# Seven drains on GpSimd: one among the experts, one in each window of the feed-forward

## The chip, the core and the metric

The kernel runs on one core of a Trainium2 chip. The metric is the device time of one execution in microseconds (us), as a median over runs. The core has five engines that matter here, each with its own stream of instructions: TensorE (PE; PEld is its weight load), VectorE (DVE), ScalarE (ACT), GpSimd (POOL) and SyncE (SP). They are tied together by semaphores alone, and the order of each stream is the order in which the kernel's code was written.

## The reference

Three layers in a row on 3072 tokens of width 384, all in float32: an attention-like scan over chunks, a mixture of 8 experts with one expert for each token, and a feed-forward with a leaky activation.

```python
def _moe_ref(x, w_gate, w_output_gate, w1, w2):
    logits = x @ w_gate
    e_idx = np.argmax(logits, axis=1)
    ...
    for e in range(E):                       # E = 8
        mask = e_idx == e
        h = np.maximum(x[mask] @ w1[e], 0.0)  # 384 -> 1024
        ye = h @ w2[e]                        # 1024 -> 384
        out[mask] = gate_w[mask, None] * eom[mask, e, None] * ye

def _moe2_ref(x, w_in, w_out):
    h = x @ w_in                              # 384 -> 2048
    g = np.maximum(0.01 * h, h)
    return (g @ w_out).astype(np.float32)     # 2048 -> 384
```

## The kernel before, in words

The scan takes roughly the first 300 us. It leaves the tokens sorted by expert in DRAM, and a small table that says for each block of 128 tokens which expert it has.

**How a float32 product is made.** Each operand of a matrix product is split into a leading part (rounded to the type fp32r) and a trailing part (the rest), and three products are summed in PSUM: leading by leading, and the two mixed ones. So each set of weights and each activation must be split before TensorE can use it.

**The experts** (about 300 to 590 us). TensorE works through the blocks of 128 tokens in a loop: layer 1 (L2060), transposes (L2036, L2070), layer 2 (L2082). The weights of an expert come in two halves, `w1` and `w2`, each 128 x 3072 elements (1536 KB), into the two halves of one staging tile `stage`. GpSimd does the splitting in `split(lot, i, ...)`: it waits until half `i` of the load has landed, and for `i == 0` also until TensorE is through with the expert before last, whose room the new weights take. It writes the leading part (L1843), waits for that on its own semaphore, writes the trailing part (L1845), waits for that too, and only then issues the load of the next lot into the same half of `stage` (L1848). There are ten lots: the eight experts, `w_out` and `w_in` of the feed-forward. Lot 0 is split elsewhere; `split` runs for lots 1 to 9. TensorE waits for the two halves of an expert's weights before that expert's first block.

**The feed-forward** (about 593 us to the end). It runs over 6 windows of 512 tokens. In a window, f counts 16 slices of the 2048 hidden elements. For each f TensorE makes the hidden slice (`ff1`, L2102, 9 matmuls), ScalarE takes a hundredth of it (L1927), VectorE the larger of the two (L1991), ScalarE its leading part (L1930), and GpSimd its trailing part (`trail(w, f)`, L1871), after which TensorE may multiply it with `w_out` (`ff2`, L2115, 12 matmuls). TensorE's order is ff1 of slice f + 2, then ff2 of slice f, so that a slice has two turns of TensorE's work in which to pass through the other engines. `act_f` has two buffers: VectorE waits for `trail` of slice f before it writes slice f + 2. After the last slice of a window GpSimd does the first two slices of the next window, and then issues four indirect DMAs that scatter the finished rows (L1877).

Of the kernel before, what the change touches and what calls it, by code (L numbers as in the profile page):

```python
# [23 lines left out]
E = 8  # L24
# [13 lines left out]
FT2 = F2 // P  # L38
# [1650 lines left out]
def experts_then_feed_forward(nc, ctx, sem, sb, bank, ident, ids, stage, masks_at, wm, wbase, w_out_r, ys, moe_w, w_in,  # L1689
# [65 lines left out]
    def at(eng, base, g, lo, hi):  # L1755
        return eng.value_load(table[0:1, bass.ds(base + g, 1)], min_val=lo, max_val=hi)
# [10 lines left out]
    def windows(eng, body):  # L1767
        for w in range(NW):
            body(w, w < NW - 1)
# [58 lines left out]
    def layers_pool(pool):  # L1828
        pool.wait_ge(s_split0, 2)
        pool.sem_inc(s_wh, 2)  # L1830
        pool.wait_ge(s_table, 1)
        pool.wait_ge(s_slots, 1)
        lots = [moe_w[e] for e in range(E)] + [w_out, w_in]

        def split(lot, i, lead, trail, done):

            u = 2 * lot + i
            half = stage[:, i * WE:(i + 1) * WE]
            pool.wait_ge(*((s_stage[i], 32) if lot == 1 else (s_more[i], 16 * (lot - 1))))
            if i == 0 and done is not None:  # L1840

                pool.wait_ge(s_p2, done)
            pool.tensor_scalar(lead, half, 1.0, 0.0, ALU.mult, ALU.add).then_inc(s_ws, 1)  # L1843
            pool.wait_ge(s_ws, u - 1)
            pool.tensor_tensor(trail, half, lead.bitcast(F32), ALU.subtract).then_inc(s_wh, 1)  # L1845
            pool.wait_ge(s_wh, u + 1)
            if lot + 1 < len(lots):
                pool.dma_start(half, lots[lot + 1][:, i * WE:(i + 1) * WE]).then_inc(s_more[i], 16)  # L1848

        def sort_ids(tiles):  # L1850
            for t in tiles:
                pool.indirect_dma_start(
                    out=sorted_ids, out_offset=bass.IndirectOffsetOnAxis(ap=slot_of[:, t:t + 1].bitcast(U32), axis=0),
                    in_=token[:, t:t + 1], in_offset=None).then_inc(s_sorted, 16)

        for e in range(1, E):
            done = at(pool, T_CUM, e - 2, 1, NBMAX) if e >= 2 else None
            for i in range(2):
                split(e, i, wm[:, e % 2, i, :], wm[:, e % 2, 2 + i, :], done)
            if 2 <= e < 2 + B:  # L1860
                sort_ids(range((e - 2) * NCH // B, (e - 1) * NCH // B))
        for i in range(2):
            split(E, i, w_out_r[:, 0, i * WE:(i + 1) * WE], w_out_r[:, 1, i * WE:(i + 1) * WE], None)
        done = at(pool, T_CUM, E - 2, 1, NBMAX)
        for i in range(2):
            split(E + 1, i, w_in_r[:, 0, i * WE:(i + 1) * WE], w_in_r[:, 1, i * WE:(i + 1) * WE], done)

        def trail(w, f):
            pool.wait_ge(s_gh, w * FT2 + f + 1)
            a = act_r[f % 4]  # L1870
            pool.tensor_tensor(a[:, 1, :], act_f[f % 2][:, :], a[:, 0, :].bitcast(F32),  # L1871
                               ALU.subtract).then_inc(s_gl, 1)

        def scatter(w):
            for j in range(TW):
                pool.wait_ge(s_o, TW * (w + 1) + j + 1)
                pool.indirect_dma_start(  # L1877
                    out=out, out_offset=bass.IndirectOffsetOnAxis(ap=ids[:, TW * w + j:TW * w + j + 1].bitcast(U32), axis=0),
                    in_=o_sb[j][:, :], in_offset=None).then_inc(s_out[j], 16)

        def body(w, more):
            for f in range(2, FT2):
                trail(w, f)
            if more:
                for f in range(2):
                    trail(w + 1, f)
            scatter(w)

        for f in range(2):
            trail(0, f)  # L1890
        pool.wait_ge(s_ids, 16)
        windows(pool, body)

    def layers_scalar(act):
# [317 lines left out]
```

## Time and profile before

| what | us |
|---|---|
| median of 3 runs | 1013.23 (1013.14 to 1015.47) |
| the profiled execution, its own time | 1014.68 |
| span of that execution, first to last instruction | 1012.7 |
| TensorE busy with matmuls | 941.1 (93% of the span) |
| GpSimd busy | 505.5 (50%) |
| ScalarE busy | 453.9 (45%) |
| VectorE busy | 415.9 (41%) |

The busy times are read first: one engine is near full, the others are at about half. A share over the whole span says little about one stage, so the stretches of the three stages are to be read apart, and for each engine what ended its idle time. The time of an instruction that does no work on data, such as a wait or a drain, isn't counted as busy; it can only be seen as idle time between its neighbours. The profiled execution's time is 1.98 us more than its span; what lies around the span is not in the profile.

### The profile page before, as it was taken

How to read it: one execution, taken by the hardware profiler on the slowest of the kernel's cores; microseconds unless marked ns; L12 is line 12 of the kernel's file. 1: busy time of each engine (PE TensorE's matmuls, PEld its weight loads, DVE VectorE, ACT ScalarE, POOL GpSimd, SP SyncE). 2: the span in 40 equal slices, each digit the busy share in tenths (PEclk: the TensorE clock that was granted, in tenths of full speed). 3: DMA queues.
4: the chain of work that ended last, by engine and by line, in shares of the span. 5: the costliest groups of instructions: out<-in, count | busy, mean ns of one | idle time of the engine just before them, and what ended most of it. 6: DMA issues, size and time to landing. Idle time of an engine off the chain costs nothing.

```text
span 1012.7 us, 17328 instructions
## 1 busy us (share of the span) xinstructions
PE 941.1 (93%) x5836; PEld 832.5 (82%) x5837; DVE 415.9 (41%) x742; ACT 453.9 (45%) x772; POOL 505.5 (50%) x429
## 2 busy tenths in 40 slices
PE   1899999999838999999999999999999999999995
PEld 0677778887736999998998989999999999999995
DVE  6698998998844233233232322212112121121110
ACT  7899888897612232232222333333333333333322
POOL 4134565565556568568839943342342433433433
PEclk9999999999978999999999999999999999999998
DMA  4542463430252343343534520010010100000000
GB/s 149 166 134 80 124 214 103 112 110 17 100 171 96 106 163 107 103 163 104 155 114 163 186 57 17 16 39 16 9 39 17 39 16 17 32 1 1 32 1 32
DMA packets 47190, 84.04 MB, mean 83 GB/s; under 512 B 23812, under 2 KB 36376, under 8 KB 44568
## 3 DMA queue, kind: packets, MB, share of 16 engines
q1 hardware_dynamic: 40984, 48.59, 16.0%
q0 software_dynamic: 6144, 34.65, 9.7%
q8 instruction: 37, 0.61, 0.3%
q14 instruction: 25, 0.20, 0.1%
HBM read 65.80 MB, written 17.38 MB: 82 GB/s over the span
## 4 chain that ended last, share of the span: by engine, by line
PE 72%; ACT 10%; issue 6%; DVE 6%; POOL 4%; SPq 1%; DMA 1%; POOLq 0%; DVEq 0%; ACTq 0%
PE bank L2102 20%; PE bank L2115 19%; PE bank L2060 11%; PE bank L2082 10%; POOL wm L1845 3%; PE bank L2070 2%; PE bank L1136 1%; PE bank L1119 1%; PE bank L1138 1%; POOL wm L1843 1%; PE bank L1096 1%; DVE neglog L848 1%; PE bank L1178 1%; PE bank L2036 1%; PE bank L1106 1%
## 5 line engine op out<-in xcount | busy, mean ns | idle before, releaser
L1871 POOL TENSOR_TENSOR act_r<-act_f,act_r 128x512 fp32r<-128x512 f32 x96 | 124.4, 1296 | 260.5 <-ACT act_r L1930 257.8
L2115 PE MATMUL bank<-w_out_r,act_r 128*128 128x384 f32 x1152 | 217.7, 337 | 0.3 <-POOL act_r L1871 0.3
L2102 PE MATMUL bank<-x,w_in_r 128*128 128x512 f32 x864 | 216.7, 395 | 0.0
L2115 PEld LDWEIGHTS bank<-w_out_r,act_r 128*128 128x128 f32 x1152 | 204.8, 188 | 8.8 <-POOL act_r L1871 0.6
L1991 DVE TENSOR_TENSOR act_f<-bank,small 128x512 f32<-128x512 f32 x96 | 66.4, 692 | 292.7 <-ACT small L1927 275.2
L2102 PEld LDWEIGHTS bank<-x,w_in_r 128*128 128x128 f32 x864 | 159.6, 188 | 29.4
L1927 ACT ACTIVATE small<-bank 128x512 f32<-128x512 f32 x96 | 57.4, 598 | 191.5 <-PE bank L2102 191.4
L2060 PE MATMUL bank<-wm,x_tr 128*128 (+1 forms) x522 | 129.1, 401 | 4.0 <-POOL wm L1845 1.7
L2082 PE MATMUL bank<-wm,h_tr 128*128 (+1 forms) x696 | 128.6, 339 | 0.7 <-DVE h_tr L1975 0.7
L2082 PEld LDWEIGHTS bank<-wm,h_tr 128*128 128x128 f32 x696 | 120.1, 188 | 1.0 <-issue 1.0
L2060 PEld LDWEIGHTS bank<-wm,x_tr 128*128 128x128 f32 x522 | 97.6, 191 | 24.8 <-issue 5.0
L1845 POOL TENSOR_TENSOR wm<-stage,wm 128x3072 fp32r<-128x3072 f32 x14 | 95.3, 6808 | 1.2
L1930 ACT ACTIVATE act_r<-act_f 128x512 fp32r<-128x512 f32 x96 | 60.7, 632 | 72.8 <-DVE act_f L1991 72.8
L1907 ACT ACTIVATE h_tr<-bank 128x512 fp32r<-128x512 f32 x58 | 31.6, 596 | 120.5 <-PE bank L2070 120.5
L1843 POOL TENSOR_SCALAR wm<-stage 128x3072 fp32r<-128x3072 f32 x14 | 38.9, 2780 | 71.3 <-PE bank L2082 56.3
L1902 ACT ACTIVATE h<-bank 128x512 f32<-128x512 f32 x58 | 31.5, 596 | 71.4 <-PE bank L2060 71.4
L1119 PE MATMUL bank<-q_t,k_t 96*128 96x128 f32 x384 | 56.2, 291 | 4.5 <-ACT q_t L696 2.7
L1981 DVE COPY y_b<-bank 128x384 f32<-128x384 f32 x29 | 16.2, 558 | 95.1 <-PE bank L2082 80.4
L1136 PE MATMUL bank<-ident,qr 128*96 128x128 f32 x192 | 46.8, 282 | 7.3 <-DVE qr L911 7.3
L1119 PEld LDWEIGHTS bank<-q_t,k_t 96*128 96x128 f32 x384 | 48.3, 197 | 6.1 <-ACT q_t L696 4.2
L1966 DVE CAST x_tr<-bank 128x384 fp32r<-128x384 f32 x30 | 16.7, 558 | 80.5 <-PE bank L2036 80.5
L1975 DVE TENSOR_TENSOR h_tr<-bank,h_tr 128x512 fp32r<-128x512 f32 x58 | 37.4, 686 | 21.3 <-ACT h_tr L1907 21.0
(193 smaller groups left out, 1378.1 us busy)
## 6 DMA issues: line engine op xcount, KB each, us to landing
stage<-moe_w POOLq DMA_DIRECT2D x12, 1536.0 KB, 7.0
qkv_in<-in_qkv SPq DMA_DIRECT2D x24, 576.0 KB, 5.5
a_in<-in_a SPq DMA_DIRECT2D x11, 768.0 KB, 5.3
stage<-moe_w SPq DMA_DIRECT2D x4, 1536.0 KB
x_b<-x_sorted SPq DMA_DIRECT2D x30, 193.0 KB
y_sorted<-y_b SPq DMA_DIRECT2D x29, 192.0 KB
xg<-y_sorted SPq DMA_DIRECT2D x24, 192.0 KB, 2.4
stage<-w_out POOLq DMA_DIRECT2D x2, 1536.0 KB, 7.1
```

The lines of the kernel that those rows point to most:

```text
L1119: last = pe.matmul(sc_bank[:, a * C:(a + 1) * C], k_t[h][:, a * C:(a + 1) * C], q_t[h][:, a * C:(a + 1) * C], start=True, stop=True)
L1136: pe.transpose(qt_bank[0:2 * D, a * C:(a + 1) * C], qr[n % 2][:, head, :, :].rearrange("p c d -> p (c d)"), ident[:, :])
L1843: pool.tensor_scalar(lead, half, 1.0, 0.0, ALU.mult, ALU.add).then_inc(s_ws, 1)
L1845: pool.tensor_tensor(trail, half, lead.bitcast(F32), ALU.subtract).then_inc(s_wh, 1)
L1871: pool.tensor_tensor(a[:, 1, :], act_f[f % 2][:, :], a[:, 0, :].bitcast(F32), ALU.subtract).then_inc(s_gl, 1)
L1927: act.activation(small[f % 2][:, :], h_bank[f % 2][:, :], ACT.Copy, scale=0.01).then_inc(s_c, 1)
L1930: act.activation(act_r[f % 4][:, 0, :], act_f[f % 2][:, :], ACT.Copy).then_inc(s_gh, 1)
L1991: dve.tensor_tensor(act_f[f % 2][:, :], h_bank[f % 2][:, :], small[f % 2][:, :], ALU.max).then_inc(s_g, 1)
L2060: last = pe.matmul(hid_bank[j][:, :], x_tr[:, xp, t * P:(t + 1) * P], wmf[:, part_of(base, wp * WE + t * F1 + j * 512, 512)], start=(t == ...
L2082: last = pe.matmul(ye_bank[:, 0:W], h_tr[:, hp, t * P:(t + 1) * P], wmf[:, part_of(base, wp * WE + t * W, W)], start=(t == 0 and n == 0), ...
L2102: last = pe.matmul(h_bank[f % 2][:, :], w_in_r[:, wp, t * F2 + f * P:t * F2 + (f + 1) * P], window_part(w, xp)[:, t, :], start=(t == 0 and ...
L2115: last = pe.matmul(o_bank[j][:, 0:W], a[:, ap, j * P:(j + 1) * P], w_out_r[:, wp, f * W:(f + 1) * W], start=(f == 0 and n == 0), stop=(f = ...
```

## The change

`drain()` puts an instruction into GpSimd's stream that holds the stream until the engine's earlier instructions have ended. It moves no data and releases nobody. The change adds seven: one in `split`, for lot 6 (the seventh expert's weights) and its second half, between the wait for the trailing part and the issue of the load of lot 7's second half; and one in each of the 6 windows, between `trail(w, 8)` and `trail(w, 9)`. In the built program GpSimd has 582 instructions for 575 before; the numbers of the other engines are the same, and nothing else changes its place. At the first drain the wait for the trailing part of the split (count 14 of its semaphore) is held by the drain now, and the load behind it has no wait of its own. The drains in the windows carry no wait on a semaphore.

```diff
@@ in split(lot, i, lead, trail, done) @@
             pool.tensor_tensor(trail, half, lead.bitcast(F32), ALU.subtract).then_inc(s_wh, 1)
             pool.wait_ge(s_wh, u + 1)
+            if lot == E - 2 and i == 1:
+                pool.drain()
             if lot + 1 < len(lots):
                 pool.dma_start(half, lots[lot + 1][:, i * WE:(i + 1) * WE]).then_inc(s_more[i], 16)
@@ in body(w, more) @@
             for f in range(2, FT2):
                 trail(w, f)
+                if f == FT2 // 2:
+                    pool.drain()
             if more:
                 for f in range(2):
                     trail(w + 1, f)
```

## Rows read from the trace of the kernel before

**Rows 1.** The page's head and first part: busy us, share, instructions.
```profile
span 1012.7 us, 17328 instructions
PE 941.1 (93%) x5836; PEld 832.5 (82%) x5837; DVE 415.9 (41%) x742; ACT 453.9 (45%) x772; POOL 505.5 (50%) x429
```

**Rows 2.** Busy time by stretch (columns in the first row), all engines.
```profile
core 0: us, PE busy (x) PEld busy (x) DVE busy (x) ACT busy (x) POOL busy (x), PEclk, DMA share, GB/s
480.00:548.00 68.00, 66.99 (x372) 61.04 (x373) 21.00 (x36) 19.13 (x36) 46.82 (x19) 1.00 0.43 133
548.00:593.00 45.00, 44.21 (x249) 40.35 (x250) 14.77 (x26) 12.50 (x25) 39.93 (x11) 1.00 0.46 158
593.00:997.00 404.00, 404.00 (x2052) 365.67 (x2051) 78.11 (x117) 135.07 (x232) 142.57 (x115) 1.00 0.07 21
```

**Rows 3.** Timeline, GpSimd, lots 6 and 7: start, duration, work [idle before <-releaser].
```profile
499.99 0.62 POOL L1848 DMA_DIRECT2D stage<-moe_w  x1 [0.30 <-POOL wm L1845]
500.65 2.77 POOL L1843 TENSOR_SCALAR wm<-stage 128x3072 fp32r<-128x3072 f32 x1
503.50 6.83 POOL L1845 TENSOR_TENSOR wm<-stage,wm 128x3072 fp32r<-128x3072 f32 x1
510.63 0.62 POOL L1848 DMA_DIRECT2D stage<-moe_w  x1 [0.30 <-POOL wm L1845]
527.28 2.77 POOL L1843 TENSOR_SCALAR wm<-stage 128x3072 fp32r<-128x3072 f32 x1 [16.04 <-PE bank L2082]
...
537.87 2.78 POOL L1843 TENSOR_SCALAR wm<-stage 128x3072 fp32r<-128x3072 f32 x1
540.73 6.80 POOL L1845 TENSOR_TENSOR wm<-stage,wm 128x3072 fp32r<-128x3072 f32 x1
```

**Rows 4.** Timeline, TensorE, first block of the last expert.
```profile
547.87 4.36 PE L2060 MATMUL bank<-wm,x_tr 128*128 x18 [0.84 <-POOL wm L1845]
```

**Rows 5.** The tile `stage`, 300 to 600 us: durations in ns min/median/max, and its loads.
```profile
L1845 POOL TENSOR_TENSOR wm<-stage,wm x14: 6789/6807/6829, 315.9 to 540.7; 128x3072 fp32r<-128x3072 f32 x14
...
DMA to landing us min/median/max: 6.5/6.9/7.9
```

**Rows 6.** Timeline, first window, around slices 8 and 9, several engines.
```profile
627.12 1.30 POOL L1871 TENSOR_TENSOR act_r<-act_f,act_r 128x512 fp32r<-128x512 f32 x1 [3.24 <-ACT act_r L1930]
...
631.31 1.30 POOL L1871 TENSOR_TENSOR act_r<-act_f,act_r 128x512 fp32r<-128x512 f32 x1 [2.89 <-ACT act_r L1930]
...
633.00 2.18 PEld L2115 LDWEIGHTS bank<-w_out_r,act_r 128*128 128x128 f32 x12
...
637.52 2.18 PEld L2115 LDWEIGHTS bank<-w_out_r,act_r 128*128 128x128 f32 x12
...
638.59 0.69 DVE L1991 TENSOR_TENSOR act_f<-bank,small 128x512 f32<-128x512 f32 x1 [1.64 <-ACT small L1927]
```

**Rows 7.** Timeline, last window, around slices 8 and 9.
```profile
968.17 1.30 POOL L1871 TENSOR_TENSOR act_r<-act_f,act_r 128x512 fp32r<-128x512 f32 x1 [2.89 <-ACT act_r L1930]
...
972.36 1.30 POOL L1871 TENSOR_TENSOR act_r<-act_f,act_r 128x512 fp32r<-128x512 f32 x1 [2.89 <-ACT act_r L1930]
...
978.24 1.83 PEld L2115 LDWEIGHTS bank<-w_out_r,act_r 128*128 128x128 f32 x10
```

**Rows 8.** Timeline, the last slice: GpSimd, then the weight load it releases.
```profile
997.48 1.28 POOL L1871 TENSOR_TENSOR act_r<-act_f,act_r 128x512 fp32r<-128x512 f32 x1 [2.89 <-ACT act_r L1930]
998.82 3.10 PEld L2115 LDWEIGHTS bank<-w_out_r,act_r 128*128 128x128 f32 x18 [0.61 <-POOL act_r L1871]
```

**Rows 9.** Timeline, GpSimd: the first window's last scatter, and the second window's slice 9.
```profile
670.86 0.96 POOL L1877 DMA_INDIRECT out<-o_sb,ids  x1 [0.30 <-issue]
...
699.65 1.30 POOL L1871 TENSOR_TENSOR act_r<-act_f,act_r 128x512 fp32r<-128x512 f32 x1 [2.89 <-ACT act_r L1930]
```

**Rows 10.** DMA issues by line: KB each, median us to landing.
```profile
out<-o_sb,ids POOLq DMA_INDIRECT x24, 2.6
```

**Rows 11.** Timeline, GpSimd in the scan: like instructions of unlike length.
```profile
267.93 0.20 POOL L551 TENSOR_TENSOR sel<-sel,whole_sum 128x4 f32<-128x4 f32 x1
268.21 3.27 POOL L552 TENSOR_TENSOR den<-sel,whole_sum 128x4 f32<-128x4 f32 x1
...
276.66 0.96 POOL L560 DMA_INDIRECT x_sorted<-x_ring,pos  x1 [0.30 <-issue]
277.92 4.02 POOL L560 DMA_INDIRECT x_sorted<-x_ring,pos  x1 [0.30 <-issue]
```

**Rows 12.** Timeline, the step from the experts to the feed-forward.
```profile
582.32 6.76 POOL L1845 TENSOR_TENSOR w_in_r<-stage,w_in_r 128x3072 fp32r<-128x3072 f32 x1
...
592.90 6.32 PE L2102 MATMUL bank<-x,w_in_r 128*128 128x512 f32 x27
```

## The prediction, made before the changed kernel was run

> **What bounds the kernel now.** I read the page's head first: TensorE is busy for 941.1 of 1012.7 us, GpSimd for 505.5 [rows 1]. Then the busy time by stretch, because a share over the span mixes three stages. In the feed-forward, from 593 to 997 us, TensorE is busy for 404.00 of 404.00 us, and GpSimd for 142.57 [rows 2]. In the two stretches of the experts behind the first new drain TensorE is idle for 68.00 - 66.99 = 1.01 us and for 45.00 - 44.21 = 0.79 us [rows 2]. So everything that comes behind the first drain, up to the last slices, is bound by TensorE, and a change that touches GpSimd alone can do two things: nothing, or make TensorE wait. The reader is to see in these rows that GpSimd's idle time in the feed-forward (404.00 - 142.57 = 261.43 us) is not a loss; it is the cover under which the drains lie.
>
> Then the timeline of GpSimd around the places of the drains, to see how long the idle time is right behind each, what ends it, and how much later GpSimd could be before TensorE noticed.
>
> **The change, part by part.** It removes nothing and moves nothing. It adds seven instructions on GpSimd that hold that stream until earlier work has ended. So its cost is one unknown, the time X that a drain takes once the work before it has ended, set against the slack at each of two kinds of place.
>
> *The drain at lot 6.* The trailing part of the split starts at 503.50 and takes 6.83 us, so it ends at 510.33; the load of lot 7's second half is issued 0.30 us later, at 510.63, since it waits for that same instruction [rows 3]. The engine is idle at that moment already, so the drain has nothing to wait out. Behind it stand the issue of the load, and then the split of lot 7, which starts at 527.28 after 16.04 us of idle time that TensorE ends: it was waiting for room, for the last block of an expert before [rows 3]. Two bounds follow. GpSimd itself gets late only if X is over 16.04 us. The load must have landed when the second half is split, at 537.87; issued at 510.63 and landing after at most 7.9 us [rows 5] it is there at 518.5, so it may be issued 19.3 us later. The smaller one decides: X up to 16.0 us costs nothing here. This place has to be checked with care because what comes behind is on the path: TensorE starts the last expert's first block at 547.87, after 0.84 us of waiting for the end of that very split [rows 4], which ends at 540.73 + 6.80 = 547.53 [rows 3]. Once the 16 us were used up, each further us would be paid in full.
>
> *The drains in the windows, six of them.* In the first window slice 8 is split from 627.12 to 628.42 [rows 6]. The drain then stands between it and the split of slice 9, which starts at 631.31 and was waiting for ScalarE for 2.89 us [rows 6]. Up to X = 2.89 us the drain only takes the place of that wait, and nothing on any engine moves. Beyond that slice 9 gets late, but TensorE needs it only at 637.52, where the weight load of its ff2 starts; slice 8's, already split before the drain, stands at 633.00 [rows 6]. From the end of a split to the weight load that it releases it takes 998.82 - (997.48 + 1.28) = 0.06 us, as the last slice shows, where TensorE did wait [rows 8]. So slice 9 may start as late as 637.52 - 0.06 - 1.30 = 636.16, which is 7.74 us behind the end of slice 8's split. VectorE, which needs the buffer of slice 9 back for slice 11, starts that at 638.59 [rows 6], later still. In the last window the same sum gives 978.24 - 0.06 - 1.30 - (968.17 + 1.30) = 7.41 us [rows 7]. The idle time ahead of slice 9 is 2.89 us in the first, the second and the last window [rows 6, 7, 9]; I take the four windows between to be like the first. So a drain costs the kernel nothing up to 7.4 us, and above it 6 times what is over.
>
> *How long is X?* No row of before shows a drain on GpSimd amid work. The nearest row is the wait of GpSimd on its own last instruction, 0.30 us, ahead of the load [rows 3]. That wait is there already at lot 6, and the drain takes it over, so there the low end is zero. A drain has no data to move, so I see no gain from it and no end below zero. The high end: were the drain also to wait for what GpSimd's queue of transfers still has in flight, it could take as long as the slowest load, 7.9 us [rows 5]. But little is in flight: at lot 6 the load of the first half was issued at 499.99 and is there by 507.9 at the latest, before 510.33 [rows 3, 5], and in the windows the last scatter, issued at 670.86 for the first of them and landing after 2.6 us, lies over 20 us ahead of the next drain, which stands just before slice 9 at 699.65 [rows 9, 10]. I take X = 0.3 us, the nearest row.
>
> The sum at X = 0.3 us: 0 at lot 6 (0.3 of 16.0), 6 x 0 in the windows (0.3 of 2.89, and of 7.4). At the high end, X = 7.9: 0 at lot 6, and 5 x (7.9 - 7.74) + (7.9 - 7.41) = 1.3 us in the windows. From the profiled execution's own time, 1014.68 us (span 1012.7 and 1.98 around it), that makes 1014.68, at most 1016.0. The profiled execution lies 1.45 us above the median of the runs, 1013.23, and within their spread of 1013.14 to 1015.47; carried over to the median the forecast is 1013.3 us.
>
> A rule that could speak against this: GpSimd's instructions run as software, and the Trainium skill (GPSIMD Engine Reference, section 2.1 Instruction dispatch) says that the first call of a freshly loaded routine pays some 6 us for loading its code, with no instruction in the profile to show it. No row here shows such a load behind a drain. If each drain led to one, slice 9 would start at 628.42 + 6 = 634.4 by that figure, still ahead of 636.16, so the estimate by the page and the estimate by the row give the same time; the page's figure only uses up most of the cover.
>
> **The rivals.**
>
> *A, slower: the drain is dear.* Should a drain on GpSimd take as long as a whole split of a half, 2.77 + 6.83 = 9.60 us [rows 3], it would pass the cover in all six windows: 5 x (9.60 - 7.74) + (9.60 - 7.41) = 11.5 us, hence 1013.23 + 11.5 = 1024.7 us. It would show as TensorE's weight load for slice 9 waiting for GpSimd, once in each window. The point from which it decides is X = 7.4 us, and 7.9 us for a loss over 0.3% is not enough: 3.04 us need 6 x 0.5, so X of about 8.2 us. For it speaks only that no row prices a drain. Against it: nothing on GpSimd that does so little takes so long; the longest of its single instructions here, with 128 x 3072 elements, takes 6.83 us [rows 3].
>
> *B, slower: a hiccup of GpSimd's stream at a bad place.* In the scan two small instructions take 3.27 and 4.02 us where their like take 0.20 and 0.96, some 3.1 us more each [rows 11]. What they are I can't read here; they may hang on where an instruction stands in the stream, and the change moves all that follow by one to seven places. In the feed-forward such a hiccup would be hidden. Between 527.28 and 547.53 it would not: TensorE waits for the end of lot 7's split, and 3.1 us there are 3.1 us in the end, 1016.3 us. At the start of the feed-forward there is 592.90 - (582.32 + 6.76) = 3.8 us between the last split and the first product [rows 12], so there it would be hidden too. Against it: the 14 trailing parts of the experts' weights take 6.789 to 6.829 us, none longer [rows 5], wherever they stand in the stream.
>
> *C, faster.* A gain needs an idle TensorE that the drains fill. Behind the first drain there are 1.01 + 0.79 us of idle time up to 593 [rows 2], and none of it is ended by something that a drain brings forward. Even all of it, 1.8 us, would be within 0.3%: 1011.4 us.
>
> *D, the drain does nothing.* If the stream holds for no time at all the forecast is the same, 1013.2 us. It can't be told from the forecast by the time, only by the gaps on GpSimd.
>
> **How the numbers follow.** The measurement can tell from no change what is over 0.3%, here 3.04 us. The forecast together with D has a chance of 0.92, C 0.02, A 0.03, and B 0.03. The predicted time is the forecast's, 1013.3 us. Its range comes from the spread of the runs before and the bounds of X: from 1012.4, a little under the lowest run, to 1015.4, where the highest run lies; the high end of X on top of the median, 1013.23 + 1.3 = 1014.5, is within. A and B lie outside and have 6 in 100. Of faster by over 0.3% I give 0.03 (C, and a shift between two measurements), of slower 0.05 (A and those of B that exceed the bound), of within 0.3% 0.92.
>
> **What would show it.** Right: the gap between the splits of slices 8 and 9 is still 2.89 us and ended by ScalarE, in all six windows; the split of lot 7 still starts when TensorE's block ends; TensorE is busy for the whole of the feed-forward. At lot 6 the gap of 0.30 us ahead of the load may grow, and its growth is X. Wrong: a gap at slice 9 over 2.89 us that ScalarE doesn't end prices the drain above the cover's first part, and TensorE waiting for GpSimd at slice 9 is rival A. A longer instruction or gap on GpSimd from 527 to 548 is rival B. The forecast falls altogether if a stage ahead of the first drain, where nothing was changed, differs between the two profiles by more than the whole difference in time: then the cause isn't in the drains' places at all.

## The result: 0.6% faster, and where it came from

| | before | changed |
|---|---|---|
| median of 9 runs, us | 1014.38 | 1010.25 |
| lowest, us | 1013.14 | 1007.71 |
| ratio (95% interval) | | 0.994 (0.9915 to 0.9966) |
| profiled execution, its own time, us | 1014.68 | 1014.22 |
| its span, us | 1012.7 | 1012.2 |

One of the nine executions of the changed kernel took 1897 us and is left out of the ratio. The quotient of the two medians is 0.996. The forecast was 1013.3 us with a range of 1012.4 to 1015.4; the time is below it, by a gain that I had given 3 in 100.

The two profiled executions differ by only 0.5 us, and that is a trap: a kernel's executions differ by some us in the scan, ahead of the change (apart from the one that is left out, the spans of the changed kernel's other executions are 1005.7 to 1010.2 us). So the two spans are cut at three points that both have: the first product of the first block of the experts (L2060, now L2064), the first product of the feed-forward (L2102, now L2106), and the end of GpSimd's last split (L1871, now L1873).

| stretch, us | before | changed | difference |
|---|---|---|---|
| start to the first block | 307.78 | 311.92 | +4.14 |
| first block to the feed-forward | 285.12 | 285.57 | +0.45 |
| feed-forward, to the end of the last split | 405.86 | 405.86 | 0.00 |
| from there to the end of the span | 13.94 | 8.85 | -5.09 |

The first row lies ahead of every drain of the change. In the eleven kernels below, none of which is changed there, that point lies anywhere from 305.18 to 309.04. The 311.92 is later still; this execution is the slowest of the changed kernel's eight, and why it was late stays open. The 0.45 us of the second row are within the spread too: in the nine kernels below that have no drain behind lot 6 among the experts, that stretch takes 284.3 to 285.8 us. The last row is the effect. No instruction was added in that stretch. The timeline of GpSimd at the end, first of before, then of the changed kernel (start, duration, line, work, [idle before]):

```profile
core 0 of [0], span 1012.7 us
...
1000.41 0.98 POOL L1877 DMA_INDIRECT out<-o_sb,ids  x1 [1.65 <-ACT o_sb L1922]
...
1004.23 0.96 POOL L1877 DMA_INDIRECT out<-o_sb,ids  x1 [0.30 <-issue]
```

```profile
core 0 of [0], span 1012.2 us
...
1005.00 0.98 POOL L1879 DMA_INDIRECT out<-o_sb,ids  x1 [1.65 <-ACT o_sb L1926]
...
1008.82 0.96 POOL L1879 DMA_INDIRECT out<-o_sb,ids  x1 [0.30 <-issue]
```

Behind the end of the last issue of a scatter there were 1012.7 - 1005.19 = 7.51 us; now there are 1012.2 - 1009.78 = 2.42 us. I call this stretch the tail. The landing doesn't fill it: a scatter lands 2.6 us behind the start of its issue [rows 10], here at 1004.23 + 2.6 = 1006.8, and that is 5.9 us before the end of the span.

What fills it is in the trace. The `--source` view of L151, the line that opens the block around all engines' streams (`with nc.Block()`), shows a drain of GpSimd in the kernel before (duration in ns, then the start of the first and of the last in us), with SyncE beside it:

```profile
core 0 of [0], span 1012.7 us
...
L151 POOLq DRAIN  x1: 9651/9651/9651, 1002.8 to 1002.8; - x1
...
L151 SPq DRAIN  x1: 7/7/7, 1007.0 to 1007.0; - x1
L151 SPq EVENT_SEMAPHORE  x1: 17/17/17, 1012.6 to 1012.6; - x1
```

The same view of the changed kernel:

```profile
core 0 of [0], span 1012.2 us
...
L151 POOLq DRAIN  x1: 4190/4190/4190, 1007.4 to 1007.4; - x1
```

A drain's record can open while the instructions ahead of it still run, so its end is what counts. In before it ends at 1002.80 + 9.65 = 1012.45, which is 7.27 us behind the last issue. SyncE is through at 1007.0 and, like the other engines, has one semaphore event left, which comes at 1012.6, behind GpSimd's drain. In the changed kernel the drain ends at 1011.58, which is 1.80 us behind the last issue and 0.2 us behind the landing of the last scatter.

Now the places of the drains. The timeline of the changed kernel at lot 6, which answers to [rows 3], and at slices 8 and 9 of the first window, which answer to [rows 6]:

```profile
507.29 6.80 POOL L1845 TENSOR_TENSOR wm<-stage,wm 128x3072 fp32r<-128x3072 f32 x1
519.54 0.62 POOL L1850 DMA_DIRECT2D stage<-moe_w  x1 [5.46 <-issue]
531.88 2.77 POOL L1843 TENSOR_SCALAR wm<-stage 128x3072 fp32r<-128x3072 f32 x1 [11.73 <-PE bank L2086]
...
631.71 1.30 POOL L1873 TENSOR_TENSOR act_r<-act_f,act_r 128x512 fp32r<-128x512 f32 x1 [3.24 <-ACT act_r L1934]
635.90 1.30 POOL L1873 TENSOR_TENSOR act_r<-act_f,act_r 128x512 fp32r<-128x512 f32 x1 [2.89 <-ACT act_r L1934]
```

The gap ahead of the load is 5.46 us for 0.30: the drain took some 5 us on an engine that had nothing left to do (its record is 4.89 us long and opens 0.03 us behind the end of the split). The next split still starts when TensorE gives up the room, after 11.73 us of idle time. The gaps ahead of slice 9 are 2.89 us in all six windows, as before; the records of those drains end 0.4 to 0.5 us behind the split of slice 8. The busy time by stretch has the feed-forward as it was, against [rows 2]:

```profile
593.00:997.00 404.00, 403.81 (x2051) 365.86 (x2052) 78.52 (x119) 133.93 (x230) 141.93 (x115) 1.00 0.07 21
```

(In this execution the feed-forward started at 597.49, so the stretch holds the last 4.5 us of the experts too.) So 5.2 us were spent under cover at lot 6, and 5.1 us were saved at the end.

### The profile page after: what moved, and what is told of

Same layout as the page of the kernel before. It is cut to its first block, busy times and chain, and to the rows that moved or that the text cites. A ratio compares the mean times of both kernels' runs of the same rounds, so it can differ in the third digit from the quotient of the medians.

```text
span 1012.2 us, 17335 instructions
## 1 busy us (share of the span) xinstructions
PE 944.0 (93%) x5836; PEld 835.1 (83%) x5837; DVE 415.1 (41%) x742; ACT 454.0 (45%) x772; POOL 505.8 (50%) x429
## 4 chain that ended last, share of the span: by engine, by line
PE 72%; ACT 9%; issue 6%; DVE 6%; POOL 4%; SPq 1%; DMA 1%; POOLq 0%; DVEq 0%; ACTq 0%
PE bank L2106 20%; PE bank L2119 19%; PE bank L2064 11%; PE bank L2086 10%; POOL wm L1845 3%; PE bank L2074 2%; PE bank L1136 1%; PE bank L1119 1%; PE bank L1096 1%; POOL wm L1843 1%; PE bank L1138 1%; DVE neglog L848 1%; PE bank L1164 1%; PE bank L1178 1%; PE bank L2040 1%
## 5 line engine op out<-in xcount | busy, mean ns | idle before, releaser
L1873 POOL TENSOR_TENSOR act_r<-act_f,act_r 128x512 fp32r<-128x512 f32 x96 | 124.4, 1296 | 260.5 <-ACT act_r L1934 258.1
L2106 PE MATMUL bank<-x,w_in_r 128*128 128x512 f32 x864 | 216.7, 395 | 0.0
L2106 PEld LDWEIGHTS bank<-x,w_in_r 128*128 128x128 f32 x864 | 159.6, 188 | 29.4
L2064 PE MATMUL bank<-wm,x_tr 128*128 (+1 forms) x522 | 129.6, 402 | 3.9 <-POOL wm L1845 1.7
L2064 PEld LDWEIGHTS bank<-wm,x_tr 128*128 128x128 f32 x522 | 97.9, 192 | 25.0 <-issue 5.0
```

The costliest lines, as they stand in the source:

```text
L2064: last = pe.matmul(hid_bank[j][:, :], x_tr[:, xp, t * P:(t + 1) * P], wmf[:, part_of(base, wp * WE + t * F1 + j * 512, 512)], start=(t == ...
L2106: last = pe.matmul(h_bank[f % 2][:, :], w_in_r[:, wp, t * F2 + f * P:t * F2 + (f + 1) * P], window_part(w, xp)[:, t, :], start=(t == 0 and ...
```

## The experiments

The program's own drain at the end of GpSimd's stream, behind the last scatter, is in both kernels. So the first idea was that a drain there is dear when none has run for long. Two theories about why came to stand against each other: **A**, it depends on the time, or on what else GpSimd has run, since the last drain (code that has to be fetched again); **B**, a drain pays for each DMA that GpSimd has issued since the last one. In before there are 88 of them: 24 scatters of the scan, 16 loads in `split`, 24 writes of the sorted ids and 24 scatters of the output.

All edits are shown against the kernel before, `...` standing for lines left out. Each run goes by the short name e1 to e11 from here on. Ratios are against runs of before on the same chip.

### One part of the change alone

`e1_lot6_only`: the first drain of the change alone.

```diff
+            if lot == E - 2 and i == 1:
+                pool.drain()
```

> Only the drain at lot 6 is kept; the six in the windows are gone. In the profile after, the gap ahead of the load was 5.46 us instead of 0.30, and from the end of the last scatter's issue to the end of the span it was 2.4 us instead of 7.5. Theory 1 (the program has a drain of its own at the end of GpSimd's stream, a drain costs some 5 us when none has run for long, and a drain shortly before makes it cheap): this drain lies 490 us before the end, with 96 splits of activations and 28 indirect DMAs between; if it is the last drain that counts, the tail is back at 7.5 us and the time at that of before (1013 to 1014 us). Theory 1b (one drain anywhere behind the scan is enough): the tail is 2.4 us and the time is that of after, about 5 us below before. Theory 2 (rival: the measured gain is a difference in the scan between runs, nothing that drains do): tail and time as in before, and so in every kernel of this set.

`e2_windows_only`: the six in the windows alone.

```diff
+                if f == FT2 // 2:
+                    pool.drain()
```

> Only the six drains in the windows are kept; lot 6 is as before. Theory 1: the tail is 2.4 us, the time about 5 us below before, as after. The first window's drain is the first for long and should cost some 5.2 us, so slice 9 of the first window starts about 5.2 us behind the end of slice 8 instead of 2.89, and later windows show 2.89; TensorE does not wait, since it has 7.4 us. Theory 1b: the same. Theory 2: no difference in time from before beyond the noise, tail 7.5 us.

`e3_last_window_only`: of these, the last alone.

```diff
+                if w == NW - 1 and f == FT2 // 2:
+                    pool.drain()
```

> One drain alone, in the last window behind slice 8, some 35 us before the end. Theory 1: the gap ahead of slice 9 of the last window grows from 2.89 to about 5.2 us, the tail falls from 7.5 to 2.4 us, and the time is about 5 us below before, as with all seven. A variant of theory 1 (it needs two or more drains to make the next one cheap) would leave the tail at 7.5 us. Theory 2: as before.

Measured, 6 runs each: e1 1009.74 us, ratio 0.9955 (0.9942 to 0.9967); e2 1010.03, ratio 0.9947 (0.9933 to 0.9961); e3 1009.16, ratio 0.9943 (0.993 to 0.9955); before 1014.41. Each part alone brings nearly the whole gain. The rival that it is a difference of the scan is out, and so is the idea that only a recent drain counts: e1's lies 490 us ahead of the end. (That the time since the last drain decides is hard to hold from here on.) The tails are 3.11, 2.12 and 2.12 us.

The gaps are the more telling. The timeline of e1 at lot 6:

```profile
514.13 0.62 POOL L1850 DMA_DIRECT2D stage<-moe_w  x1 [5.46 <-issue]
```

That of e2, slices 9 and 10 of the first window, and that of e3 in the last window:

```profile
634.21 1.29 POOL L1871 TENSOR_TENSOR act_r<-act_f,act_r 128x512 fp32r<-128x512 f32 x1 [5.42 <-issue]
635.88 1.29 POOL L1871 TENSOR_TENSOR act_r<-act_f,act_r 128x512 fp32r<-128x512 f32 x1 [0.37 <-ACT act_r L1932]
```

```profile
976.92 2.54 POOL L1871 TENSOR_TENSOR act_r<-act_f,act_r 128x512 fp32r<-128x512 f32 x2 [7.05 <-ACT act_r L1932]
```

In e3 I had expected about 5.2 us. The drain took 7.05, and there are 84 DMAs before it, 20 more than the 64 before e2's: 1.63 us for 20. TensorE didn't notice either: from the first product of the feed-forward to the end of the last split it is 405.86 us in all three, within 0.01.

### A drain behind every half

`e4_every_half`: the drain in `split` without a condition, 18 in all, none in the windows.

```diff
             pool.wait_ge(s_wh, u + 1)
+            pool.drain()
```

> A drain behind every split of a half, lots 1 to 9 (18 drains), ahead of each load; none in the windows. Each gap ahead of a load prices one drain: 0.30 us is the gap without. Between the two halves of a lot lie one issue of a load and two arithmetic instructions; between lots 2 to 5 and the next one lie also six indirect DMAs and a load of a register from the table. Theory 1 as a matter of code that GpSimd has to fetch again once other routines have pushed it out: the first drain costs about 5.2 us, the others little, and those after indirect DMAs perhaps 5 us again. A rival (a drain has to work off what has gathered since the last one, such as the bookkeeping of the transfers that GpSimd issued): the cost follows the number of DMAs since the last drain, greatest at the first (24 indirect DMAs of the scan), middling after six, least after one.

Its timeline at the loads of lots 1 (both halves) and 3 (both halves):

```profile
324.13 0.63 POOL L1849 DMA_DIRECT2D stage<-moe_w  x1 [2.66 <-issue]
335.17 0.61 POOL L1849 DMA_DIRECT2D stage<-moe_w  x1 [0.68 <-POOL wm L1845]
...
393.27 0.61 POOL L1849 DMA_DIRECT2D stage<-moe_w  x1 [1.20 <-issue]
404.28 0.60 POOL L1849 DMA_DIRECT2D stage<-moe_w  x1 [0.68 <-POOL wm L1845]
```

The first gap is 2.66 us with 24 DMAs before it, not 5.2; with 7 since the last drain (a load and six writes of ids) the gap is 1.20, with one 0.66 to 0.68. That is 0.087 us for each of six, and 0.086 for each of the 17 between 7 and 24. Theory A expected about 5.2 us at the first; the number of DMAs orders all gaps seen so far. (There was one execution of this kernel, 1011.67 us. Its tail is 2.87 us, but from the first block to the feed-forward it takes 288.03 us instead of some 285: eighteen drains among the experts are not all under cover.)

### The last drain far from the end, and at the wrong place

`e6_lot1_only`: one drain, behind the first half of lot 1.

```diff
+            if lot == 1 and i == 0:
+                pool.drain()
```

> One drain alone, behind the first half of lot 1. Theory B (a drain pays for the DMAs that GpSimd issued since the last drain, about 0.08 us each): 24 indirect DMAs lie before it, so its gap is 2.66 us as in the run with a drain at every half; 64 lie between it and the program's own drain at the end (16 loads, 24 and 24 indirect). From the last issue of a scatter to the span's end it took 7.5 us with 88, 3.1 with 28, and 2.1 to 2.4 with 4, so 0.073 us for each between the first two: about 5.7 us with 64, and the time 1.8 us below before (ratio 0.998). Theory A with one drain anywhere being enough: that tail under 3.1 us and the time about 5 us below (ratio 0.995). Theory A by elapsed time (the last drain 690 us before the end against 490 with lot 6 alone): between these two, with no number of its own.

Measured: 1012.30 us against 1014.37, ratio 0.9983 (0.9973 to 0.9993), 12 runs; gap 2.67, tail 1011.8 - 1006.28 = 5.52 us. Theory B's numbers were 0.998 and 5.7. (The expectation counts 28 DMAs behind the drain of e1; it is 29: 5 loads and 24 scatters.)

`e7_before_last_scatter`: one drain, behind the last split of all, ahead of the last four scatters.

```diff
+                if w == NW - 1 and f == FT2 - 1:
+                    pool.drain()
```

> One drain alone, between the last split of all and the four last scatters. Theory B: it pays for 84 DMAs, about 7.05 us as in the last window, but here on the path: the first of the last scatters starts about 7.1 us behind the end of the last split instead of 1.65, 5.4 us later; the tail behind the scatters falls from 7.5 to between 2.1 and 2.4 us, 5.2 less; the time is that of before within 0.5 us (ratio 0.9995 to 1.0005). So the gain would be a matter of where the cost lies, not of drains. If drains saved something by themselves, the ratio would be about 0.995 here too.

Its timeline at the end:

```profile
core 0 of [0], span 1011.5 us
...
995.67 1.28 POOL L1871 TENSOR_TENSOR act_r<-act_f,act_r 128x512 fp32r<-128x512 f32 x1 [2.88 <-ACT act_r L1932]
1004.65 0.98 POOL L1877 DMA_INDIRECT out<-o_sb,ids  x1 [7.70 <-issue]
...
1008.47 0.96 POOL L1877 DMA_INDIRECT out<-o_sb,ids  x1 [0.30 <-issue]
```

The scatter comes 7.70 us behind the split instead of 1.65, and the tail is 2.07 us: +6.05 and -5.44. Measured: 1015.68 us against 1014.37, ratio 1.002 (1.0007 to 1.0034), 12 runs. I had expected no change within 0.5 us, and it is slower. The scatter comes 0.6 us later than I had reckoned (7.70 for 7.1); that is about the lower end of the interval, 0.7 us, and what the rest is stays open. The drain itself took no longer than in e3. Its record, by the line of the drain, first here, then in e3:

```profile
L1885 POOLq DRAIN  x1: 8279/8279/8279, 995.6 to 995.6; - x1
```

```profile
L1885 POOLq DRAIN  x1: 8294/8294/8294, 968.5 to 968.5; - x1
```

It ends 6.96 us behind the split ahead of it in both; the scatter is issued 0.74 us behind that end, where e3's split starts 0.09 us behind it. The kind of thing is as expected: the same work is done, only in the open. A drain saves nothing by itself.

### More DMAs

`e8_more_dmas_one_row` and `e9_more_dmas_128_rows`: the drain of e3, and 24 more DMAs issued by GpSimd, which write to a spare tensor (1 row of 4 bytes; in e9 128 rows). SyncE waits for them at the end, with its waits for the scatters. `e10_more_dmas_no_drain`: the DMAs of e8, and no drain.

```diff
...
+                if w < 4 and f in (4, 6, 8, 10, 12, 14):
+                    k = 6 * w + f // 2 - 2
+                    pool.dma_start(spare[k, 0:1, :], pos[0:1, 0:1]).then_inc(s_sorted, 16)
+                if w == NW - 1 and f == FT2 // 2:   # not in e10
+                    pool.drain()
```

> The one drain in the last window, as in the run with it alone (gap ahead of slice 9 there 7.05 us with 84 DMAs since the start), and 24 more DMAs issued by GpSimd in the first four windows, six in each, that write one row of 4 bytes each to a spare tensor. Theory B by number of DMAs: 24 x 0.0815 = 2.0 us more, gap about 9.0 us. Theory B by rows or descriptors moved: no more than 0.1 us more. Theory A (time or other code since the last drain): 7.05 us.

> As the one before, with 128 rows of 4 bytes in each of the 24 added DMAs. By number of DMAs: about 9.0 us again. By rows: the 24 x 128 rows are as many as those of 24 scatters of 128 rows; the 20 scatters between the first window's gap of 5.42 and the last's of 7.05 cost 1.63 us, so again about 9.0 us. With the one-row kernel this tells number from rows: both 9.0, number; 7.05 and 9.0, rows.

The timelines at slice 9 of the last window, e8, then e9:

```profile
976.08 2.51 POOL L1874 TENSOR_TENSOR act_r<-act_f,act_r 128x512 fp32r<-128x512 f32 x2 [9.01 <-issue]
```

```profile
976.11 2.51 POOL L1874 TENSOR_TENSOR act_r<-act_f,act_r 128x512 fp32r<-128x512 f32 x2 [9.01 <-issue]
```

(One execution of each, 1008.32 and 1008.40 us.) The gap is 9.01 us in both, where 9.0 had been worked out from the number: 1.96 us over e3 for 24 DMAs, 0.082 us each, and not a hundredth of a us for 127 rows more in each. Time and other work since the start are as in e3. Theory A is out, and so is a cost by rows. These gaps also pass the cover that the prediction had reckoned for a drain in the last window, 7.41 us: the feed-forward up to the last split now takes 407.27 us (e8) instead of 405.86, so 1.41 us are paid, where 9.01 - 7.41 gives 1.60.

> No drain is added at all; GpSimd issues 24 more DMAs of one row of 4 bytes in the first four windows. Theory B: the program's own drain at the end pays for 112 instead of 88, so the tail from the last scatter's issue to the end of the span grows from 7.5 us by 24 x 0.0815 = 2.0 to about 9.5 us, and the time is 2 us above before (ratio 1.002), although the added DMAs themselves lie under TensorE's work, some 50 us and more before the end. Rival (the tail of before is something else that a drain happens to shorten, not the program's own drain counting DMAs): tail 7.5 us, ratio 1.000.

Measured: 1015.70 us against 1014.47, ratio 1.002 (1.0007 to 1.0034), 11 runs. The timeline of GpSimd's last scatter in it:

```profile
core 0 of [0], span 1014.0 us
...
1003.60 0.96 POOL L1880 DMA_INDIRECT out<-o_sb,ids  x1 [0.30 <-issue]
```

The tail is 1014.0 - 1004.56 = 9.44 us; expected were 9.5. The kernel gets slower by DMAs that lie over 100 us before its end, and the feed-forward itself is unchanged (405.84 us). This ties the tail to the program's own drain: no other drain stands behind a DMA in this kernel, and its record has grown from 9.65 to 11.61 us, by 1.96 us:

```profile
L151 POOLq DRAIN  x1: 11614/11614/11614, 1002.2 to 1002.2; - x1
```

### What a drain costs by itself, and the cover behind lot 7

`e5_eight_in_a_row`: at lot 6, eight drains instead of one.

```diff
+            if lot == E - 2 and i == 1:
+                for _ in range(8):
+                    pool.drain()
```

> Eight drains in a row at lot 6, none elsewhere. With one the gap was 5.46 us, with 59 DMAs issued by GpSimd before it. Theory B (a drain pays about 0.08 us for each DMA that GpSimd issued since the last drain, and little for itself): the seven behind the first have none to pay for, so the gap is 5.46 us plus seven times a fixed cost, at most 0.3 us each (with one DMA since the last drain the gap was 0.68, 0.38 over that without a drain), hence 5.6 to 7.6 us. If each drain paid for all DMAs of the program so far, drained or not, the gap would be over 40 us.

Its timeline at that load:

```profile
514.50 0.61 POOL L1851 DMA_DIRECT2D stage<-moe_w  x1 [5.90 <-issue]
```

The gap is 5.90 us for 5.46 with one: (5.90 - 5.46) / 7 = 0.06 us for a drain that has no DMA to pay for (the records of the seven are 0.034 us long). A drain does not pay again for DMAs that an earlier one has paid for. (One execution, 1008.82 us.)

`e11_lot7_only`: one drain, one lot later than in e1 (`lot == E - 1 and i == 1`).

> One drain alone, one lot later: behind the second half of lot 7, ahead of the load of w_out's second half. 61 DMAs lie before it, so the gap is 5.46 + 2 x 0.08 = 5.6 us, 5.3 more than 0.30. GpSimd has no idle time from there to the end of lot 9 to take it up, so lots 8 and 9 are 5.3 us late; the last split then ends 5.3 us later, and TensorE, which had 3.8 us to spare there, starts the feed-forward 1.5 us later (by the end of the last split). The tail has 27 DMAs to pay for: about 3.0 us instead of 7.5. Sum: 1.5 - 4.5 = -3.0 us, ratio about 0.997, against 0.9955 with the drain at lot 6. Should the place not matter, the ratio is 0.9955 here too.

Its timeline, GpSimd at the load and TensorE at the start of the feed-forward:

```profile
551.60 0.59 POOL L1850 DMA_DIRECT2D stage<-w_out  x1 [5.61 <-issue]
...
593.15 6.38 PE L2104 MATMUL bank<-x,w_in_r 128*128 128x512 f32 x27 [1.67 <-POOL w_in_r L1845]
```

Measured: 1011.25 us against 1014.47, ratio 0.9972 (0.9963 to 0.9981), 11 runs; tail 2.99 us. The gap is 5.61 for 5.6 expected, TensorE waits for GpSimd for 1.67 us for 1.5, and the ratio is the 0.997 of the sum. So the cover is real, and its end is where the timeline of before puts it.

### All of it in one table

| drain at | DMAs since the last drain | gap or tail, us | from the end of the work ahead to the end of the drain's record, us |
|---|---|---|---|
| a load (gap 0.30 without): e4, e4, e4, e1, e11 | 1, 7, 24, 59, 61 | 0.68, 1.20, 2.66, 5.46, 5.61 | 0.16, 0.66, 2.07, 4.93, 5.09 |
| a split in a window: e2, e3, e8 | 64, 84, 108 | 5.42, 7.05, 9.01 | 5.32, 6.96, 8.92 |
| ahead of the last scatters: e7 | 84 | 7.70 | 6.96 |
| the program's end (tail): changed and e3, e4, e11, e1 | 4, 24, 27, 29 | 2.42 and 2.12, 2.87, 2.99, 3.11 | 1.80, 2.62, 2.76, 2.83 |
| the same: e6, before, e10 | 64, 88, 112 | 5.52, 7.51, 9.44 | 5.30, 7.27, 9.23 |

From 1 to 61 DMAs at a load the gap grows by 4.93 us, 0.082 for each; in the windows by 0.082; in the tail from 64 to 112 by 0.082. The last column puts the places on one line: with 64 DMAs it has 5.32 us in a window and 5.30 at the end. At the program's end the cost flattens out below some 30: 1.80 us with 4 DMAs, where a window of the changed kernel has 0.4. There the last scatter is still under way, since it lands 1.6 us behind the end of its issue. The drain ends 0.20, 1.03, 1.16 and 1.24 us behind that landing with 4, 24, 27 and 29 DMAs, so it looks as if a part of its work waited for the landing; no run was made to test that. So the change takes the program's own drain from 88 DMAs to 4.

No version beats the changed one: e2 and e3 are as fast within the intervals, e3 with one drain instead of seven. Of the tail of 2.1 us that they leave, the last scatter's landing takes 1.6 us.

## Why the prediction was wrong

**The step that failed is the first: "a change that touches GpSimd alone can do two things: nothing, or make TensorE wait"**, and with it "I see no gain from it and no end below zero". It holds up to the last slices, as the prediction says itself, and then the prediction leaves the rest out. Rival C sums the idle time of TensorE "behind the first drain" up to 593 us and with the feed-forward's none; the 13.94 us from the last split to the end of the span are in no sum. In them GpSimd is what is waited for. Its last scatter has landed at 1004.23 + 2.6 = 1006.8 [rows 10], and the span ends 5.9 us later. Those 5.9 us that nothing explained were the lower bound that the sum should have had, and would have made the low end about 1007.3 us, which holds the measured 1010.25. The reason given against a gain was that a drain has no data to move. That it may do work that another drain would do later was not considered, though the program ends with one. The trace of before even had a price: the document said ahead of the prediction that a drain can only be seen as idle time between its neighbours, but the view of L151 has its record, 9.65 us long. The measured gain passes all of rival C, whose 1.8 us already lay outside the stated range.

**X, the time of a drain, was mis-sized**: 0.3 us was taken, from a wait on GpSimd's own last instruction, and the drain at lot 6 made that gap 5.16 us longer (4.89 us is its record). The high end of 7.9 us was worked out from a different mechanism, transfers in flight; it holds for this change, but only by accident: at lot 6 nothing was in flight that could last so long, and with 108 DMAs the gap was 9.01. Something of that mechanism shows only at the program's end, where the drain with 4 DMAs ends 0.2 us behind the last landing.

**The cover was right.** Lot 6 had 16.0 us, of which the drain used 5.2: the split of lot 7 still starts when TensorE gives up the room. A window has 7.4 to 7.7 us: 7.05 us in e3 cost nothing, 9.01 in e8 cost 1.41. Behind lot 7, 3.8 us [rows 12]: e11 is late by 1.67. That the drains would leave the gaps at slice 9 at 2.89 us came out in all six windows, though for a reason that the prediction didn't have. With the drain at lot 6 ahead of them, each pays for only four or five DMAs.

**The rivals.** A (the drain is dear) had the right suspicion about size, but took each of the six as equally dear, and looked only at what it costs where it stands. B (a hiccup) didn't come: GpSimd's splits from lot 7 on are as before. C named the right sign and no place. D is refuted by the gap of 5.46 us.

**The rule that was weighed** gave a number near the drain's, and for the wrong reason. The first drain's gap is 5.46 us. The Trainium skill (GPSIMD Engine Reference, section 2.1 Instruction dispatch) has some 6 us for the first call of a freshly loaded routine. But the first drain of e4 shows 2.66 us and that of e8 9.01: the number of DMAs decides, and the page's figure doesn't. The Trainium skill (PSUM — Partial Sum Buffer, section Engine vs sequencer instructions) also says that a drain waits for the engine to go fully idle. Here the wait for the last instruction was over and the drain took 5 us more; the measurement goes beyond the rule.

What stays open is what GpSimd does for 0.08 us a DMA. The Trainium skill (DMA: Bandwidth & Descriptors, section SWDGE vs HWDGE vs iDMA) states that for the DMAs that GpSimd issues the descriptors are computed by software on one of its cores. That some record of each DMA is put in order when GpSimd drains is a guess from there, and no run here looks into it.

## What to carry to other kernels

Cut the span at points that both traces share, and include the stretch behind the last instruction: the time from the landing of the last transfer to the end is idle time that somebody owns. Ask the trace for the line of the program's own drain too, since the timeline leaves it out. On GpSimd count the DMAs that it issues: here each left some 0.08 us for the next drain (some 0.04 at the program's end, where the last landing was waited out as well), and the program ends with one. So in a kernel with many of them it is worth trying one drain late in the kernel, with few DMAs behind it, at a place where the slack is more than its own price (here 5.2 to 7.1 us). e7 shows the same drain without cover, and e11 one with too little. An instruction that seems to do nothing may take over work that is otherwise done later, in the open.

## What the runs showed of the hardware that was not expected

- A drain on GpSimd costs 0.082 us for each DMA that GpSimd issued since the last drain (slopes at loads, in windows and at the end, from 64 DMAs on, agree), whether it is a load of 1536 KB, an indirect write of ids or a write of one row; 0.06 us with none.
- It costs this also when the transfers have long landed: in e8 the 24 added ones were issued over 100 us before.
- The drain itself takes the same wherever it stands: with 84 DMAs it ends 6.96 us behind the work ahead of it in e3 and in e7. What follows starts 0.09 us later if it is a split (e3), 0.53 if it is a load (e1), 0.74 if it is a scatter (e7).
- At the program's end, with 4 DMAs to pay for, the drain ends 0.20 to 0.21 us behind the landing of the last scatter, in all six kernels that have it so.
- Executions differ by some us in the scan, whose code is the same in all thirteen kernels: the first block of the experts starts anywhere from 305.2 to 311.9 us in their profiles, more than the whole effect of the change; single profiles can only be compared stretch by stretch.
